# Order of work at the joints of an attention, gated feed-forward and routed feed-forward kernel

## What is computed

```python
rel = pos[:, None] - pos[None, :]
Dmat = np.where(rel >= 0, gamma[:, None, None] ** rel, 0.0)
x = np.matmul(scale * np.matmul(q, k.T) * Dmat, v)          # per batch and head
xn = x / np.sqrt(np.mean(x * x, -1, keepdims=True) + 1e-06) * rms_g
g = xn @ w_gate
y = (g / (1 + np.exp(-g)) * (xn @ w_val)) @ w_out
e = np.argmax(y @ w_gate2, axis=1)
out[e == i] = gate * eom * (np.maximum(y[e == i] @ w1[i], 0) @ w2[i])
```

## Time and profile before

| | us |
|---|---|
| runs | 882.36 (881.67 to 883.47, three runs) |
| the profiled execution | 893.08 |
| its span, first to last instruction | 891.1 |
| TensorE busy | 803.2 (90%) |
| VectorE busy | 519.7 (58%) |
| ScalarE busy | 425.7 (48%) |
| GpSimd busy | 450.9 (51%) |
| mean granted clock of TensorE | 0.964 |

### The profile page before, as it was taken

One profiled execution on the slowest core, in us unless ns is written; L12 is line 12 of the kernel. 1 busy time (PEld: TensorE's weight loads), 2 busy tenths in 40 slices (PEclk: granted clock), 3 DMA queues, 4 the chain that ended last, 5 costly groups with the idle time before them and its releaser, 6 DMA issues.

```text
span 891.1 us, 14837 instructions
## 1 busy us (share of the span) xinstructions
PE 803.2 (90%) x5053; PEld 706.5 (79%) x5053; DVE 519.7 (58%) x798; ACT 425.7 (48%) x815; POOL 450.9 (51%) x384
## 2 busy tenths in 40 slices
PE   7997688877899999789999999972999999999995
PEld 6886578776679999667999978842888888888884
DVE  3577678998535888653688632351455454554553
ACT  3564464444445555354655423521355454455453
POOL 3568976667754888664688523156112112222221
PEclk9998899999999999799999999987999999999998
DMA  9982012113121223212124012311545545556553
GB/s 317 318 285 86 24 49 70 48 48 95 48 60 36 72 88 125 76 55 60 29 76 143 28 47 67 123 37 32 172 144 163 185 155 169 177 160 173 161 169 103
DMA packets 48362, 99.65 MB, mean 112 GB/s; under 512 B 7490, under 2 KB 8644, under 8 KB 48295
## 3 DMA queue, kind: packets, MB, share of 16 engines
q1 hardware_dynamic: 42934, 87.40, 31.1%
q0 software_dynamic: 4944, 10.96, 4.2%
q10 hardware_dynamic: 432, 0.63, 0.2%
HBM read 89.50 MB, written 10.40 MB: 112 GB/s over the span
## 4 chain that ended last, share of the span: by engine, by line
PE 70%; POOL 10%; DVE 9%; issue 5%; ACT 3%; another core or an unknown queue 2%; DMA 1%; SPq 0%; POOLq 0%; ACTq 0%; DVEq 0%
PE banks L1392 7%; PE banks L1394 6%; PE banks L1393 6%; PE banks L1446 5%; PE banks L1579 5%; PE banks L1580 5%; PE banks L1448 5%; PE banks L1447 5%; PE banks L1581 5%; PE banks L1379 4%; PE banks L1380 4%; PE banks L1381 4%; POOL AL L493 3%; POOL AL L487 2%
## 5 line engine op out<-in xcount | busy, mean ns | idle before, releaser
L1392 PE MATMUL banks<-BH,AH 128*128 128x384 f32 x504 | 175.4, 348 | 29.7 <-DVE g L779 13.3
L1393 PE MATMUL banks<-BL,AH 128*128 128x384 f32 x504 | 171.2, 340 | 0.0
L1394 PE MATMUL banks<-BH,AL 128*128 128x384 f32 x504 | 171.1, 339 | 0.0
L1392 PEld LDWEIGHTS banks<-BH,AH 128*128 128x128 f32 x504 | 96.0, 191 | 41.5 <-DVE g L779 16.5
L809 DVE TENSOR_TENSOR hidL<-hid,hidH 128x384 fp32r<-128x384 f32 x72 | 55.8, 780 | 91.9 <-ACT hidH L1086 91.9
L493 POOL TENSOR_TENSOR AL<-s_ab,AH 128x1024 fp32r<-128x1024 f32 x36 | 94.7, 2631 | 12.5 <-ACT AH L1064 12.3
L1446 PE MATMUL banks<-dH,hidH 128*128 128x512 f32 x216 | 87.4, 405 | 12.9 <-DVE hidL L809 12.9
L1394 PEld LDWEIGHTS banks<-BH,AL 128*128 128x128 f32 x504 | 96.4, 191 | 0.0
L1393 PEld LDWEIGHTS banks<-BL,AH 128*128 128x128 f32 x504 | 96.2, 191 | 0.0
L505 POOL TENSOR_TENSOR dL<-wraw,dH 128x512 fp32r<-128x512 f32 x36 | 49.0, 1362 | 85.6 <-ACT dH L1079 85.6
L1579 PE MATMUL banks<-wH,h2H 128*112 128x512 f32 x192 | 77.7, 405 | 14.4 <-DVE h2L L963 14.4
(11 more groups left out here) (179 smaller groups left out, 1723.2 us busy)
## 6 DMA issues: line engine op xcount, KB each, us to landing
wraw<-w_moe SPq DMA_DIRECT2D x168, 256.0 KB, 2.7
wraw<-w_moe SPq DMA_DIRECT2D x36, 512.0 KB, 3.6
vr<-v_rows SPq DMA_DIRECT2D x15, 320.0 KB, 4.6
qt<-q_t SPq DMA_DIRECT2D x16, 288.0 KB, 4.6
y_rows<-y_sb SPq DMA_DIRECT2D x6, 768.0 KB, 6.0
kt<-k_t SPq DMA_DIRECT2D x15, 288.0 KB, 4.3
kr<-k_rows SPq DMA_DIRECT2D x16, 256.0 KB, 3.2
mask<-c_mask SPq DMA_DIRECT2D x4, 160.0 KB, 5.5
```

The lines of the kernel that those rows point to most:

```text
L1392: mm(to, wh, bh, start=first and k == 0, stop=False, skip_group_check=True)
L1393: mm(to, wh, bl, start=False, stop=False, skip_group_check=True)
L1394: i = mm(to, wl, bh, start=False, stop=k == 1, skip_group_check=True)
```

## The change

Attention: the statistics of batch 2 are made one unit later (after unit 13), each batch's into its own place; the roots of batches 2 and 3 get buffers of their own (late). For the first two inner rows all four sums of weights are made by VectorE (sums_four), and for the combinations T3 and NT4 of block 0 VectorE also makes the low half (low_first). The preparation of the first products is put into other units.

Entry of block 0: TensorE's order was m2, m5, last statistics, m1; now it is m2, last statistics, m1, m5 (in the other blocks m2, m1, m5). ScalarE takes the roots of the last batch before it loads the sigmoid's table, where it did so in step 1.

Steps: tasks are spread over two phases, 11 in the steps of block 0 (one in each, between the two hidden products) and 11 in its output rows. The first output row of a block is split in two halves, put before m7 and m4 of the last step, with its hidden halves made in the last two steps. In the output rows ScalarE makes the weights' high half between the two hidden ones; the four sums of the next block go to rows 0, 1, 4 and 6, and its low halves to rows 0, 1, 2, 3, 5, 6 and 7. Three of the six bank copies move into the next block's first steps.

Routing: of the fifteen later scatters the first five are issued at once, the others in groups of 3, 3, 2 and 2, for each of which GpSimd waits for another up product of TensorE.

```diff
@@ -59,6 +59,7 @@
 EARLY = 3
+CLOCKED = (8, 11, 14, 16)
...
@@ -311,6 +321,13 @@
+        DVE_LOW = (T3, NT4)
+
+        def lows(blk, b):
+
+            return blk * 7 - (len(DVE_LOW) if blk > 0 else 0) + b + 1
+
+        DOWN_B = {0: B21, 1: B11, 2: B22, 3: T1, 5: T2, 6: T3, 7: NT4}
...
@@ -516,41 +533,38 @@
                 if u > 0 and (u - 1) % PAIRS > 0:
                     add_squares(u - 1)
+                if u == 9:
+                    low_a(0)
                 if u == 10:
-                    sums_a(0)
...
                 if u == 11:
                     low_b(0, B11)
-                    low_a(0)
                 if u == 12:
...
                 if u == 13:
+                    low_b(0, B22)
+                if u == 14:
+                    low_b(0, T1)
+                if u == 15:
                     low_b22(0)
-                if u == 14:
-                    low_b(0, B22)
-                    sums_a(1)
-                    low_a(1)
-                if u == 15:
-                    low_b(0, T1)
             low_b(0, T2)
+            low_a(1)
             low_S(1)
-            low_b(0, T3)
             low_b22(1)
-            low_b(0, NT4)
             for blk in range(BLOCKS):
...
                 for f in range(F1):
+                    if f >= F1 - 2:
+                        low_down(n0 + f - F1 + 2)
...
                     low_b22(n0 + f + 2)
-                    if f >= F1 - 2:
-                        low_down(n0 + f - F1 + 2)
                 for f in range(F1):
                     if f < F1 - 2:
                         low_down(n0 + f + 2)
-                    if blk + 1 < BLOCKS and f < 7:
-                        low_b(blk + 1, f)
+                    if blk + 1 < BLOCKS and f in DOWN_B:
+                        low_b(blk + 1, DOWN_B[f])
...
@@ -595,7 +609,9 @@
             pool.sem_inc(s_issued, 1)
-            scatter_records(range(EARLY, TILES))
+            for f, (lo, hi) in enumerate(zip((EARLY,) + CLOCKED, CLOCKED + (TILES,))):
+                wait(pool, s_up, f)
+                scatter_records(range(lo, hi))
...
@@ -726,6 +744,21 @@
+
+            def sums_four(n):
+
+                sums_two(n)
+                r = wraw[:, n % 2, :]
+                dve.wait_ge(s_Sd, 4 * n + 1)
+                V.tensor_tensor(s_ab[:, 1, :], s_ab[:, 0, :], r[:, 0:HK], ALU.subtract).then_inc(s_Sd, 1)
+                dve.wait_ge(s_Sd, 4 * n + 3)
+                V.tensor_tensor(s_ab[:, 3, :], r[:, HK:2 * HK], s_ab[:, 1, :], ALU.subtract).then_inc(s_Sd, 1)
+
+            def low_first(b):
+
+                dve.wait_ge(s_BH, b + 1)
+                V.tensor_tensor(BL[:, b], t3[:] if b == T3 else x_part(0, b), BH[:, b].bitcast(F32),
+                                ALU.subtract).then_inc(s_BLd, 1)
...
@@ -746,18 +779,15 @@
                 if u == 12:
...
                 if u == 9:
-                    sums_two(0)
+                    sums_four(0)
                 if u == 13:
-                    sums_two(1)
...
                 if u == 14:
-                    root(2, HALVE, TIMES)
-                    normalise(2, 0)
+                    sums_b(0, T2)
                 if u == 15:
-                    sums_b(0, T2)
                     sums_b(0, NT4)
-                    root(2, FIX)
+                    sums_four(1)
...
@@ -788,19 +825,18 @@
                 V.tensor_tensor(hv[:, 1:2, :], g1[:], sig[:, 1:2, :], ALU.mult).then_inc(s_hv1, 1)
+                run(between)
...
                 V.tensor_tensor(hid[:, f:f + 1, HALF:BLOCK], hv[:, 1:2, :], v1[:], ALU.mult).then_inc(s_h1, 1)
-                for task in more[0:1]:
-                    task()
+                run(then)
...
                 V.tensor_tensor(hid[:, f:f + 1, 0:HALF], hv[:, 0:1, :], x, ALU.mult).then_inc(s_h0, 1)
-                for task in more[1:]:
-                    task()
+                run(last)
...
@@ -815,24 +851,26 @@
             def root_task(b, no):
...
-            LATER = ([norm_task(2, k) for k in range(1, KD)] + [norm_task(3, k) for k in range(KD)] + [root_task(3, i) for i in range(3)]
-                     + [norm_task(4, k) for k in range(KD)] + [norm_task(5, k) for k in range(KD)])
+            def low_task(m):
+                return lambda: low_hidden(m)
+
+            IN_UP = [root_task(2, i) for i in range(3)] + [norm_task(q, k) for q in (2, 3) for k in range(KD)]
+            IN_DOWN = [root_task(3, i) for i in range(3)] + [norm_task(q, k) for q in (4, 5) for k in range(KD)]
+            DOWN_T = {0: T3, 1: T1, 4: T2, 6: NT4}
             for blk in range(BLOCKS):
...
                 for f in range(F1):
-                    hidden(n0 + f, LATER[2 * f:2 * f + 2] if blk == 0 else ())
-                low_hidden(2 * n0)
-                low_hidden(2 * n0 + 1)
+                    hidden(n0 + f, [low_task(2 * n0 + 1)] if f == F1 - 1 else (), IN_UP[f:f + 1] if blk == 0 else (),
+                           [low_task(2 * n0)] if f == F1 - 2 else ())
                 for f in range(F1):
-                    if blk + 1 < BLOCKS and f == 0:
-                        sums_b(blk + 1, T3)
-                        sums_b(blk + 1, T1)
-                    if blk + 1 < BLOCKS and f == 4:
-                        sums_b(blk + 1, T2)
-                        sums_b(blk + 1, NT4)
                     if f < F1 - 1:
                         low_hidden(2 * (n0 + f + 1))
+                    if blk + 1 < BLOCKS and f in DOWN_T:
+                        sums_b(blk + 1, DOWN_T[f])
+                    if f < F1 - 1:
                         low_hidden(2 * (n0 + f + 1) + 1)
+                    if blk == 0:
+                        run(IN_DOWN[f:f + 1])
...
@@ -1107,40 +1152,43 @@
-            def evacuate_y(blk, a):
+            def take_y(blk, a, j):
                 act.wait_ge(s_down, blk * (2 * F1) + 2 * (F1 - 1) + a + 1)
-                for j in range(TPH):
-                    S.activation(y_sb[:, (2 * blk + a) * TPH + j, :], banks[:, DOWN[a][j], :], ACT.Copy).then_inc(s_y, 1)
+                S.activation(y_sb[:, (2 * blk + a) * TPH + j, :], banks[:, DOWN[a][j], :], ACT.Copy).then_inc(s_y, 1)
...
             def up_step(n):
...
+                blk, f = n // F1, n % F1
...
                 gate(n, 0)
-                if n == 0:
-                    high_b(0, NT4)
...
                 gate(n, 1)
-                if n % F1 < F1 - 1:
+                if f < F1 - 1:
...
                 high_S(n + 2)
-                if n % F1 < F1 - 1:
+                if f < F1 - 1:
...
                 high_b22(n + 2)
-                if n == 1:
-                    mean_square(BATCH - 1)
-                if n % F1 >= F1 - 2:
-                    high_down(n - F1 + 2)
+                if blk > 0 and f < TPH:
+                    take_y(blk - 1, 1, f)
+                if f == F1 - 3:
+                    high_down(n - f)
+                if f == F1 - 2:
+                    high_hidden(2 * (n - f))
+                    high_hidden(2 * (n - f) + 1)
+                    high_down(n - f + 1)
...
                 if f < F1 - 1:
                     high_hidden(2 * (n + 1))
-                    high_hidden(2 * (n + 1) + 1)
                 if f < F1 - 2:
                     high_down(n + 2)
-                if blk + 1 < BLOCKS and f < 7:
-                    high_b(blk + 1, f)
+                if f < F1 - 1:
+                    high_hidden(2 * (n + 1) + 1)
+                if blk + 1 < BLOCKS and f in DOWN_B:
+                    high_b(blk + 1, DOWN_B[f])
...
@@ -1158,30 +1206,33 @@
                 if u + 2 < UNITS:
                     decay_k(u + 2)
-                if u in (5, 9, 13):
+                if u in (5, 9, 14):
                     mean_square((u - 5) // PAIRS)
+                if u == 9:
+                    high_a(0)
                 if u == 10:
                     high_b(0, B21)
-                    high_a(0)
                 if u == 11:
                     high_b(0, B11)
+                if u == 12:
                     high_S(0)
-                if u == 12:
+                if u == 13:
+                    high_b(0, B22)
                     high_b22(0)
-                if u == 13:
+                if u == 14:
+                    high_b(0, T1)
                     high_a(1)
-                    high_b(0, B22)
-                if u == 14:
+                if u == 15:
+                    high_b(0, T2)
+                    high_b(0, T3)
                     high_b22(1)
-                    high_b(0, T1)
-                if u == 15:
-                    high_S(1)
+            evacuate_last()
+            copy_y(0)
+            high_b(0, NT4)
+            high_S(1)
+            mean_square(BATCH - 1)
+            copy_m5(0)
             S.activation(one_sig[:], eps[:, 0:1], ACT.Sigmoid)
-            evacuate_last()
-            high_b(0, T2)
-            copy_y(0)
-            copy_m5(0)
-            high_b(0, T3)
...
@@ -1189,13 +1240,10 @@
                 for f in range(F1):
                     up_step(n0 + f)
```

(70 more changed lines are left out.)

55 lines of the change are left out of this document (32 added, 23 removed).

## The result

The changed kernel took 892.15 us in the median (889.47 to 895.04, 4 runs) beside 882.91 us (881.67 to 886.45) of the kernel before: a ratio of 1.0088, 95% interval 1.006 to 1.0116. It is slower by 0.9% where 832.7 us was forecast. Its profiled execution took 889.47 us with a span of 887.6 us.

The account below looks back on a forecast made before the run. TensorE was taken to set the end everywhere, so its gaps could be won. Terms of -9.0, -13.0, -6.7, -10.0, -4.0 and -7.0 summed to -49.7 us, from the median 882.36 to 832.7, range 818 to 856.

Parts of the forecast that it names:

- I expect no gap in blocks 1 and 2: Output products of blocks 1 and 2: TensorE would have no idle time, with terms of -10.0 and -4.0 us including last steps.
- The rule of the port: VectorE and GpSimd take turns at their shared port, each holding it for a whole instruction.
- Block 0's steps: Block 0's ten steps: nine of 8.4 us and a tenth of 9.4, 85.0 for 98.04, -13.0 us.
- rival (b): Attention, steps, output stages: turns at the port eat the spreading, steps of 8.7 us and more, -29 us, 853; chance 0.17.
- over 9.2 us: Block 0's steps: one taking longer than this, or under 7.7 us, would show the prediction wrong.
- Attention: Before block 0: TensorE's stop of about 5.8 us for batch 2's statistics goes, later VectorE costs some back; 4.2 us gained.
- The entry: Entry of block 0: a 3.5 us wait for ScalarE's copy replaces the old wait; 20.83 us becomes some 16, -4.8.
- The last steps: End of each block's steps: early halves of output products close gaps of 3 to 6.5 us in three places.
- The first steps of a block: Block 1's steps: 1.6 us added, 0.55 for a copy right on its product, the rest low halves in steps 10 and 11.
- The scatters: Behind the routing: a first group of five frees TensorE earlier, -12.7, with 6 given back by later groups; -7 us.
- rival (a): Behind the routing: the scatter term is nil, as the hold isn't the burst's or belongs to the profiled execution; 839.7 us, 0.20.
- The rival with a slower kernel: Record scatters: a fixed hold of 14.4 us for each burst, paid for each of five groups; 897 us, chance 0.03.

Follow-up runs that it names:

- a_order: The changed kernel with ScalarE making both hidden high halves before the weight's high half again in the output rows; 875.45 us beside 883.96.
- b_order: The kernel before with only ScalarE's new order in the output rows, the weight's high half between the two hidden ones; 908.75 us, ratio 1.0286.
- a_yield: The changed kernel with GpSimd's low half of the next weight held back until VectorE has made both hidden low halves; 872.16 us beside 893.28.
- b_again: The kernel before, unchanged, profiled anew; profiled execution 882.64 us, median 884.16 us in its group of runs.
- o_tasks: a_order with block 0's eleven normalising tasks behind VectorE's two sums instead of between the two hidden products; 861.57 us beside 893.33 of the kernel before.
- a_again: The changed kernel, unchanged, run again beside the unchanged kernel before; 893.28 us, ratio 0.9975.
- o_whole: a_order with the first inner row's output products in one piece behind the last step again; 880.12 us beside 893.33 of the kernel before.
- b_again2: The kernel before, unchanged, run once more beside the unchanged changed kernel; 894.14 us.

## Why the prediction was wrong

- **The first step that failed** is the sentence "Now ScalarE makes the weight's high half between the two hidden ones, so GpSimd starts its 1.3 us two microseconds earlier". The weight's high half writes a buffer that the row before must have left, with both its halves: it waits for the same event as the second hidden high half. So GpSimd starts 0.71 us behind that event (531.72 to 532.43 us in after) where it started 1.13 behind it (520.32 to 521.45 in a_order): 0.4 us earlier, not two. VectorE's low half, which now waits for a later copy, starts 1.08 us behind the event instead of 0.56, so that GpSimd comes from 0.57 us behind it to 0.37 ahead of it. "I expect no gap in blocks 1 and 2" came from this and from counting durations, not turns: the rows got 18.8 us longer. a_order, b_order and a_yield show it from three sides. The rule of the port had been read from the trace two paragraphs earlier, and was not applied to this pair.
- **Block 0's steps**, -13.0 forecast, -3.0 measured. The price of a task was taken as at most 1.3 us on top of a loop of 7.4 to 8.0. A step with one task takes 9.45 us now; with two it took 8.97 to 11.05 in b_again, and about as long as now (9.31 to 9.59) in four of the nine steps. VectorE comes 0.07 us behind GpSimd's low half of the sums and loses that whole turn (2.7 us) as well. It is rival (b), at a higher price than it named, and the sign "over 9.2 us" came true. Spreading the tasks was worth little, their place was worth 15 us of the steps (o_tasks).
- **Attention**, -4.2 forecast, -0.9 measured, which is less than executions differ among themselves: block 0 begins at 86.8 to 90.0 us in six profiles with the attention of before and at 86.7 to 89.2 in eight with that of after. The stop for the statistics of batch 2 is gone, but VectorE's four sums stand in one unit and three of them wait their turn at the port: a new stop of 3.25 us and the lower clock behind it (1.72 us for 1.16). The prediction spread these waits over the units and took 2 us as the least gain.
- **The entry** was right in its mechanism: the wait (2.83 us, 3.5 forecast) is on ScalarE's copy behind the high halves of the sums, as said. That the stage took 16.12 us for some 16 forecast is in part luck: the same kernel with the same wait (2.82 us) took 18.87 in a_again, at a granted clock of 0.82 in the entry for 1.00 in after.
- **The last steps**, right in their mechanism and too large: from the last step to row 1 there are 9.5 us of products (30 of 384 columns, 18 of 512), 28.6 in the three blocks, and nothing else was to be left. After takes 39.6, b_again 47.6. The halves alone are worth 3.7 in the three blocks (o_whole); a half waits for its hidden low half on VectorE, and TensorE still waits for the gates.
- **The first steps of a block** got 0.7 us longer, forecast 0.55, and step 10 of block 1 by 1.1, as said.
- **The scatters**: against the profiled execution of before the term was nearly right (-7 forecast, 6 to 7 where the burst is held), and releases of up to 3 us behind later groups were foreseen. It was then subtracted from a median of runs that had no hold. The 10.7 us between the profile and the median stood in the text, with rival (a) beside it at 0.20, and should have been read as the hold itself: b_again's profile, without it, is 10.4 us shorter. In runs like those the term is +1 to +2.
- **Signs.** The rival with a slower kernel was a hold of 14.4 us in each group of scatters; none of over 3.0 occurs. What made the kernel slower was in no rival. The 56.5 us between forecast and stage table are: the output rows 21.1 (162.8 us for the 141.7 that the prediction's prices give), the last steps 11, the tasks 10, the scatters 8.9, attention and entry 3.6, and 1.9 of small ones.

## What to carry to other kernels

Where two engines take whole turns at a port, an instruction that arrives a tenth of a microsecond late pays the other's full length, so ask of each reordering which of the two will be issued first, and hold back the one that nobody waits for (here one wait of GpSimd gave 21 us). Before costing a moved step at "earlier", look up what it waits for: if its wait ends with that of the step it is put ahead of, it can only delay. When the profiled execution is longer than the timed runs and holds a wait that nothing in it explains, price a change with and without that wait before subtracting it from the median of the runs.

## What the runs showed of the hardware

- Beside a burst of 15 indirect scatters from GpSimd, a semaphore release from TensorE reached ScalarE 15.0 and 15.4 us late in two profiles of the same kernel (before, b_again2) and at once in a third (b_again); it goes with the time of the execution (893.08 and 893.65 us held, 882.64 not). In the two groups of runs with 893 to 894 us the releases beside paced scatters (5, 3, 3, 2 and 2) were late by at most 3.0 us.
- VectorE and GpSimd do the same work in block 0's steps in 7.7 us (o_tasks), where the hidden product is issued 0.6 us ahead of GpSimd's low half and takes 1.07, and in 9.45 us (after), where the task stands elsewhere, the product comes 0.07 us behind and takes 2.74.
- The entry of block 0 ran at a granted clock of 1.00 in one execution of the changed kernel (after, 16.12 us) and of 0.82 in another (a_again, 18.87 us), with a wait of the same length before its last products (2.83 and 2.82 us).
